# First tile of an attention and two-layer kernel: loads in pieces, no filler matmuls between blocks, another softmax for group 0

## The chip, the cores and the metric

The kernel runs on one core of one Trainium2 chip. The metric is the time of one execution on the device in microseconds (us). TensorE (PE in the profile) multiplies matrices, PEld is its weight load, VectorE is DVE, ScalarE is ACT, GpSimd is POOL, and SyncE (SP) issues the DMAs that bring data from HBM into on-chip memory.

## The reference

The input is a set of attention heads (4 batches, 8 heads, 768 positions, head size 64), each position attending to its own chunk of 32, 16 positions to the left, 8 to the right and 8 memory slots. The result goes through two feed-forward layers.

```python
def _attn_ref(q, k, v, mem_k, mem_v):
    for c in range(nc):                      # 24 chunks of 32
        scores = scale * np.matmul(q_c, k_full.transpose(0, 1, 3, 2))
        scores = scores - np.max(scores, axis=-1, keepdims=True)
        a = np.exp(scores)
        a = a / (np.sum(a, axis=-1, keepdims=True) + 1e-09)
        out[:, :, c_start:c_end] = np.matmul(a, v_full)

def _moe_ref(x, w_in, w_out):                # x is 3072 x 512, d_ff 2048
    h = x @ w_in
    g = np.maximum(0.01 * h, h)
    return g @ w_out

def _moe2_ref(x, w_in, w_out, a, b):
    h = x @ w_in
    P = a[0] + a[1]*h + a[2]*h**2 + a[3]*h**3
    Q = 1.0 + abs(b[0])*abs(h) + abs(b[1])*h**2
    return (P / (Q + 1e-06)) @ w_out
```

All of it is float32. The kernel splits each float32 matrix into a high and a low part and forms three products.

## The kernel before

The 3072 rows are cut into 8 tiles of 384, and each tile into 3 groups of 128. Phase A is attention and the first layer for all tiles, phase B the second layer. In phase A the attention of the next tile is woven into the matmuls of the present one. The first tile has no tile before it, so its three groups run alone at the start of the program, in an order written out by hand for each engine. This stretch, up to `first_gemm1`, is what the diff touches.

For one group, TensorE does `scores` (32 small matmuls, each of which the trace records as two, so 64), then VectorE takes maxima, ScalarE the exponential, TensorE four transpositions (`transpose_probs`), ScalarE copies them out of PSUM (`save_probs_t`), and TensorE does `values` (again 64 records). VectorE then divides by the row sums (`normalise`) and transposes in blocks (`turn_heads`), ScalarE rounds to the high part (`save_heads`) and VectorE forms the low part (`save_heads_low`). `first_gemm1` waits for the high parts of all three groups.

Two ways of doing the softmax exist. `first_exp` (line 653) reads scores from PSUM in eight pieces, each with its own bias, and lets ScalarE sum up each piece; VectorE only gives the maxima and a product for the bias (`first_maxima`). `shift_scores` with `exp_scores` (lines 788 and 649), used in the loop, has VectorE subtract the maxima over all 512 elements, ScalarE take one exponential, and VectorE sum (`sum_rows`).

`keep_warm(n)` issues n matmuls of 384 columns on a zeroed buffer whose result nobody reads. SyncE's program is a list: the q and k part and the v part of groups 0 to 2, the identity, four slices of the first layer's weights, then group 3, then more weights. `load_qk` for a later group waits for `scores_ready`, `load_v` for `heads_ready`, `load_raw` for `w_ready`, which GpSimd raises when it has split a slice (`split_half`). The four `raw` buffers are a ring. The semaphore `heads_ready` counts groups whose `values` are done.

Of the kernel before, what the change touches and what calls it, by code (L numbers as in the profile page):

```python
# [29 lines left out]
ALU = mybir.AluOpType  # L30
# [15 lines left out]
GPT = TILE // P  # L46
# [30 lines left out]
def build(nc, groups, weights, coef, ident_in, out):  # L77
# [166 lines left out]
    def ring(c):  # L244
        return c if c < 3 else c % 2

    def loads(g, c):

        if c < 3:
            return 16  # L250
        return (g - c % 2) * 8 + (16 if c % 2 else 0)

    with nc.Block() as block:

        @block.sync
        def _(sp):

            def load_qk(g, c):
                src = groups[bass.ds(g, 1), :, :].rearrange("a p n -> (a p) n")
                if c >= 3:  # L260
                    sp.wait_ge(scores_ready, g - 1)
                sp.dma_start(grp[ring(c)][:, 0:Q_W + K_W], src[:, 0:Q_W + K_W]).then_inc(qk_loaded[ring(c)], 16)

            def load_v(g, c):
                src = groups[bass.ds(g, 1), :, :].rearrange("a p n -> (a p) n")
                if c >= 3:
                    sp.wait_ge(heads_ready, g - 1)
                sp.dma_start(grp[ring(c)][:, Q_W + K_W:GRP_W], src[:, Q_W + K_W:GRP_W]
                             ).then_inc(v_loaded[ring(c)], 16)

            def load_group(g, c):
                load_qk(g, c)
                load_v(g, c)

            def load_raw(j, r, first=False):

                if not first:
                    sp.wait_ge(w_ready, j - RAW + 1)
                sp.dma_start(raw[:, r, :], weights[bass.ds(j, 1), :, :].rearrange("a p n -> (a p) n")
                             ).then_inc(raw_loaded[r], 16)  # L280
# [39 lines left out]
            sp.sem_inc(y_stored, 1)  # L320


            load_qk(0, 0)
            load_qk(1, 1)
            load_qk(2, 2)
            sp.dma_start(ident[:, :], ident_in).then_inc(ident_loaded, 16)
            for c in range(3):
                load_v(c, c)
            for j in range(RAW):
                load_raw(j, j, first=True)  # L330
            sp.dma_start(cf[:, 0:6], coef).then_inc(coef_loaded, 16)
            load_group(3, 3)
            for j in range(RAW, 2 * RAW):
                load_raw(j, j - RAW)
            load_raw(8, 0)
            load_raw(9, 1)
            load_group(4, 4)
# [100 lines left out]
        def _(pe):  # L438
# [1 line left out]


            def wait_scores(g, c, own_place=False):
                pe.wait_ge(qk_loaded[ring(c)], loads(g, c))
                if not own_place:
                    pe.wait_ge(x_ready, g)

# [16 lines left out]
                last.then_inc(transposed, 1)  # L463

            def wait_values(g, c):
                pe.wait_ge(v_loaded[ring(c)], loads(g, c))
                pe.wait_ge(probs_t_ready, g + 1)

            def values(c, at):
# [12 lines left out]
            def keep_warm(count):  # L482

                for _ in range(count):
                    nc.tensor.matmul(psum[:, H_BANKS[1], 0:TILE], g_hi[:, 0, 0:P], g_hi[:, 0, :], start=True, stop=True)  # L485
# [126 lines left out]
            pe.wait_ge(zeros_ready, 1)  # L612
            keep_warm(13)
            first_scores(0)
            keep_warm(4)
            first_scores(1)
            keep_warm(5)
            first_scores(2)
            keep_warm(2)
            pe.wait_ge(ident_loaded, 16)  # L620
            transpose_probs(0, first_att[0])
            keep_warm(2)
            transpose_probs(1, first_att[1])
            first_values(0)
            first_values(1)
            keep_warm(2)
            transpose_probs(2, first_att[2])
            keep_warm(2)
            first_values(2)
            keep_warm(8)  # L630
            first_gemm1()
            for f in range(1, LAG):
                gemm1(f, f, 0, False)
# [14 lines left out]
        def _(act):  # L648
# [109 lines left out]


            assert GPT == 3  # L760
            first_exp(0, first_att[0])
            first_exp(1, first_att[1])
            save_probs_t(0, first_att[0])
            save_probs_t(1, first_att[1])
# [22 lines left out]
        def _(dve):  # L787
# [15 lines left out]
                                        at.max_v.unsqueeze(3).broadcast_to([P, SETS, CPG, KEYS]),  # L803
                                        ALU.subtract).then_inc(shifted, 1)

            def first_maxima(g, gi, at):

                dve.wait_ge(scores_ready, g + 1)
                if gi == 0:
                    edge = at.scores[:, :, 0, N_MEM:N_MEM + LEFT]  # L810
                    nc.vector.tensor_scalar(edge, edge, NEG, None, ALU.add).then_inc(masked, 1)
                    dve.wait_ge(masked, 1)
                nc.vector.tensor_reduce(at.max_v, at.scores, AX.X, ALU.max).then_inc(maxima_ready, 1)
                dve.wait_ge(maxima_ready, g + 1)
                nc.vector.tensor_scalar(at.safe, at.st[:, 0, :], -SCALE, None, ALU.mult).then_inc(shifted, 1)
# [28 lines left out]
            def turn_heads(g, at):  # L844

                dve.wait_ge(normalised, g + 1)
                nc.vector.transpose(at.heads_t, at.probs).then_inc(turned, 1)
# [102 lines left out]
            nc.vector.memset(g_hi[:, 0, :].bitcast(F32), 0.0).then_inc(zeros_ready, 1)  # L950
            nc.vector.memset(cf[:, 7:8], Q_ONE).then_inc(consts_ready, 1)
            dve.sem_inc(yl_saved, KT)
            for g in range(GPT):
                first_maxima(g, g, first_att[g])
            first_inverses(0, first_att[0])
            first_inverses(1, first_att[1])
            for g in (0, 1):
                normalise(g, first_att[g])
                turn_heads(g, first_att[g])
            first_inverses(2, first_att[2])  # L960
            save_heads_low(0, 0, 0, first_att[0])
            normalise(2, first_att[2])
# [67 lines left out]
```

## Time and profile before

| | us |
|---|---|
| median of 3 runs | 1157.43 |
| lowest, highest | 1156.36, 1158.45 |
| profiled execution, its own time | 1156.13 |
| its span, first to last instruction | 1154.4 |
| TensorE matmuls busy | 1140.4 |
| mean granted TensorE clock | 0.997 |

The span is what the trace covers; 1.73 us of the profiled execution lie outside it. Lines of the trace carry the numbers of this kernel. "Idle before" is the time an engine stood still before an instruction, with what released it; "issue" there means that it waited for nothing that the profile shows. All positions in the trace are counted from the start of the span.

### The profile page before, as it was taken

What the parts mean: (1) busy time and instruction counts of PE and PEld (TensorE: products, weight loads), DVE (VectorE), ACT (ScalarE), POOL (GpSimd) and SP (SyncE); (2) the same over time, 40 slices, a digit from 0 to 9 for tenths busy, and PEclk for the clock granted to TensorE, in tenths of its full rate; (3) what the DMA queues carried; (4) which work ended last, traced back from release to release, by engine and by line L of the source; (5) the groups of instructions that cost most, each with busy time, mean ns of one, the idle gap of its engine ahead of it and who ended that gap; (6) DMA issues with size and microseconds to landing.
All of it is one profiled execution on the core that took longest, in us unless ns stands there. A gap on an engine that the chain in (4) does not pass through costs nothing.

```text
span 1154.4 us, 22877 instructions
## 1 busy us (share of the span) xinstructions
PE 1140.4 (99%) x8966; PEld 1068.7 (93%) x8966; DVE 742.3 (64%) x1384; ACT 568.5 (49%) x1199; POOL 133.3 (12%) x132
## 2 busy tenths in 40 slices
PE   7999999999999999999999999999999999999998
PEld 6999999999999999999999999999999999999996
DVE  4654444544445354444327888888888888888886
ACT  4333223323232232322227676676767667676765
POOL 4981130211202111100000000000000000000000
PEclk8999999999999999999999999999999999999999
DMA  7652534425525254210687010020201002020000
GB/s 267 208 176 87 165 136 141 144 74 183 175 94 186 78 183 157 100 56 2 264 291 246 2 54 30 1 83 1 83 1 66 18 1 83 1 83 1 28 1 28
DMA packets 43016, 114.78 MB, mean 99 GB/s; under 512 B 4896, under 2 KB 5024, under 8 KB 42912
## 3 DMA queue, kind: packets, MB, share of 16 engines
q1 hardware_dynamic: 42912, 113.33, 28.4%
q8 instruction: 72, 1.18, 0.4%
q14 instruction: 32, 0.26, 0.1%
HBM read 77.66 MB, written 35.65 MB: 98 GB/s over the span
## 4 chain that ended last, share of the span: by engine, by line
PE 97%; DVE 1%; ACT 1%; issue 1%; DVEq 0%
PE psum L504 15%; PE psum L506 15%; PE psum L505 15%; PE psum L519 8%; PE psum L538 8%; PE psum L539 8%; PE psum L521 8%; PE psum L520 8%; PE psum L537 7%; PE psum L476 2%; PE psum L453 1%; PE psum L461 1%; PE psum L485 1%; DVE g_lo L862 0%; DVE scratch L859 0%
## 5 line engine op out<-in xcount | busy, mean ns | idle before, releaser
L504 PE MATMUL psum<-x_hi,w_hi 128*128 128x384 f32 x1020 | 342.4, 336 | 1.0 <-DVE x_lo L853 0.8
L506 PE MATMUL psum<-x_hi,w_lo 128*128 128x384 f32 x1020 | 342.6, 336 | 0.0
L505 PE MATMUL psum<-x_lo,w_hi 128*128 128x384 f32 x1020 | 341.6, 335 | 0.0
L859 DVE TENSOR_TENSOR scratch<-psum,scratch 128x384 f32<-128x384 f32 x128 | 71.3, 557 | 235.4 <-ACT scratch L680 234.7
L680 ACT ACTIVATE scratch<-psum 128x384 f32<-128x384 f32 x128 | 62.9, 492 | 277.4 <-PE psum L506 273.5
L504 PEld LDWEIGHTS psum<-x_hi,w_hi 128*128 128x128 f32 x1020 | 191.5, 188 | 7.5 <-issue 1.6
L505 PEld LDWEIGHTS psum<-x_lo,w_hi 128*128 128x128 f32 x1020 | 191.5, 188 | 5.4
L506 PEld LDWEIGHTS psum<-x_hi,w_lo 128*128 128x128 f32 x1020 | 191.4, 188 | 0.0
L519 PE MATMUL psum<-g_hi,w_hi 128*128 128x384 f32 x512 | 177.5, 347 | 0.0
L521 PE MATMUL psum<-g_hi,w_lo 128*128 128x384 f32 x512 | 171.2, 334 | 0.0
L520 PE MATMUL psum<-g_lo,w_hi 128*128 128x384 f32 x512 | 171.2, 334 | 0.0
L539 PE MATMUL psum<-w_hi,g_lo 128*128 128x512 f32 x384 | 152.0, 396 | 0.0
L538 PE MATMUL psum<-w_lo,g_hi 128*128 128x512 f32 x384 | 151.7, 395 | 0.0
L537 PE MATMUL psum<-w_hi,g_hi 128*128 128x512 f32 x384 | 149.5, 389 | 1.5 <-DVE g_lo L868 1.5
L700 ACT ACTIVATE scratch<-psum,cf 128x384 f32<-128x384 f32 x128 | 74.7, 584 | 150.8 <-PE psum L506 150.8
L862 DVE TENSOR_TENSOR g_lo<-scratch,g_hi 128x384 fp32r<-128x384 f32 x128 | 83.7, 654 | 74.2 <-ACT g_hi L686 74.2
L882 DVE SCALAR_TENSOR_TENSOR scratch<-scratch,cf 128x384 f32<-128x384 f32 x128 | 79.1, 618 | 77.8 <-ACT scratch L701 77.8
L686 ACT CAST g_hi<-scratch 128x384 fp32r<-128x384 f32 x128 | 65.7, 513 | 81.8 <-DVE scratch L859 81.8
L519 PEld LDWEIGHTS psum<-g_hi,w_hi 128*128 128x128 f32 x512 | 96.1, 188 | 3.8
L520 PEld LDWEIGHTS psum<-g_lo,w_hi 128*128 128x128 f32 x512 | 96.2, 188 | 0.0
L521 PEld LDWEIGHTS psum<-g_hi,w_lo 128*128 128x128 f32 x512 | 96.1, 188 | 0.0
L539 PEld LDWEIGHTS psum<-w_hi,g_lo 128*128 128x128 f32 x384 | 72.0, 187 | 15.4
(78 smaller groups left out, 1421.7 us busy)
## 6 DMA issues: line engine op xcount, KB each, us to landing
scratch<-groups_in SPq DMA_DIRECT2D x23, 768.0 KB, 4.5
raw<-weights_in SPq DMA_DIRECT2D x64, 256.0 KB, 4.1
scratch<-groups_in SPq DMA_DIRECT2D x23, 512.0 KB, 4.1
w_hi_scratch<-w_high SPq DMA_DIRECT2D x32, 256.0 KB, 4.1
w_lo_scratch<-raw SPq DMA_DIRECT2D x32, 256.0 KB, 4.2
w_hi<-w_hi_scratch SPq DMA_DIRECT2D x32, 256.0 KB, 3.7
w_lo<-w_lo_scratch SPq DMA_DIRECT2D x32, 256.0 KB, 4.6
x_hi_scratch<-x_hi SPq DMA_DIRECT2D x8, 768.0 KB, 3.3
```

The lines of the kernel that those rows point to most:

```text
L504: nc.tensor.matmul(bank, hi, x_hi[:, b, k, :], start=(k == 0), stop=False)
L505: nc.tensor.matmul(bank, hi, x_lo[:, b, k, :], start=False, stop=False)
L506: last = nc.tensor.matmul(bank, lo, x_hi[:, b, k, :], start=False, stop=(k == KT - 1))
L519: nc.tensor.matmul(bank, hi, g_hi[:, f % G_RING, :], start=(f == 0), stop=False)
L520: nc.tensor.matmul(bank, hi, g_lo[:, f % G_RING, :], start=False, stop=False)
L521: last = nc.tensor.matmul(bank, lo, g_hi[:, f % G_RING, :], start=False, stop=(f == NF - 1))
L537: nc.tensor.matmul(bank, hi, w_hi[:, f, 1, :], start=(f == 0), stop=False)
L538: nc.tensor.matmul(bank, hi, w_lo[:, f, 1, :], start=False, stop=False)
L539: last = nc.tensor.matmul(bank, lo, w_hi[:, f, 1, :], start=False, stop=(f == NF - 1))
L700: nc.scalar.activation(absb, h, ACT.Abs, scale=cf[:, 4:5])
L862: nc.vector.tensor_tensor(g_lo[:, f % G_RING, :], leaky[f % 2], g_hi[:, f % G_RING, :].bitcast(F32), ALU.subtract).then_inc(g_lo_ready, 1)
L882: nc.vector.scalar_tensor_tensor(quad[c], h2, cf[:, 6:7], absb, ALU.mult, ALU.add).then_inc(quad_ready, 1)
```

## The change

Three things change in the first tile. The loads of groups 0 to 2 are cut into pieces of 512 columns (2 KB per partition, 256 KB each), and the wait counts of `qk_loaded` and `v_loaded` grow with the number of pieces; slices 4 and 5 of the weights wait until two groups have their `values` done, and group 3, the coefficients and slices 6 and 7 until all three have. The `keep_warm` calls between the attention blocks are gone (17 matmuls), the first one of 13 stays and the last one has 9 instead of 8. Group 0 takes its softmax the way of the loop: difference on VectorE, one exponential on ScalarE, sums on VectorE; the inverses and `normalise` steps are listed anew.

```diff
-    def loads(g, c):
+    def loads(g, c, pieces):
         if c < 3:
-            return 16
-        return (g - c % 2) * 8 + (16 if c % 2 else 0)
+            return 16 * pieces
+        return 16 * (pieces - 1) + (g - c % 2) * 8 + (16 if c % 2 else 0)
...
-            load_qk(0, 0)
-            load_qk(1, 1)
-            load_qk(2, 2)
+            def load_first(c, lo, hi, loaded):
+                for at in range(lo, hi, 512):
+                    sp.dma_start(grp[c][:, at:at + 512], groups[c, :, at:at + 512]).then_inc(loaded[c], 16)
+            for c in range(3):
+                load_first(c, 0, Q_W + K_W, qk_loaded)
             sp.dma_start(ident[:, :], ident_in).then_inc(ident_loaded, 16)
             for c in range(3):
-                load_v(c, c)
+                load_first(c, Q_W + K_W, GRP_W, v_loaded)
             for j in range(RAW):
                 load_raw(j, j, first=True)
+            sp.wait_ge(heads_ready, 2)
+            load_raw(4, 0)
+            load_raw(5, 1)
+            sp.wait_ge(heads_ready, GPT)
+            load_group(3, 3)
             sp.dma_start(cf[:, 0:6], coef).then_inc(coef_loaded, 16)
-            load_group(3, 3)
-            for j in range(RAW, 2 * RAW):
-                load_raw(j, j - RAW)
+            load_raw(6, 2)
+            load_raw(7, 3)
...
             keep_warm(13)
             first_scores(0)
-            keep_warm(4)
             first_scores(1)
-            keep_warm(5)
             first_scores(2)
-            keep_warm(2)
             pe.wait_ge(ident_loaded, 16)
             transpose_probs(0, first_att[0])
-            keep_warm(2)
             transpose_probs(1, first_att[1])
             first_values(0)
             first_values(1)
-            keep_warm(2)
             transpose_probs(2, first_att[2])
-            keep_warm(2)
             first_values(2)
-            keep_warm(8)
+            keep_warm(9)
             first_gemm1()
...
-            first_exp(0, first_att[0])
+            exp_scores(0, first_att[0])
             first_exp(1, first_att[1])
...
-            for g in range(GPT):
-                first_maxima(g, g, first_att[g])
-            first_inverses(0, first_att[0])
+            shift_scores(0, 0, 0, 0, first_att[0])
+            first_maxima(1, first_att[1])
+            sum_rows(0, first_att[0])
+            first_maxima(2, first_att[2])
             first_inverses(1, first_att[1])
```

TensorE, from the start of the program to the first matmul of the first layer: the kernel before, then the changed one.

```order
L485 MATMUL psum<-g_hi 128x384 x12
L453 MATMUL psum<-scratch 32x64 [waits qk_loaded0]
L453 MATMUL psum<-scratch 32x64 x31
L485 MATMUL psum<-g_hi 128x384 x4
L453 MATMUL psum<-scratch 32x64 [waits qk_loaded1]
L453 MATMUL psum<-scratch 32x64 x31
L485 MATMUL psum<-g_hi 128x384 x5
L453 MATMUL psum<-spare 32x64 [waits qk_loaded2]
L453 MATMUL psum<-spare 32x64 x31
L485 MATMUL psum<-g_hi 128x384 x2
L461 MATMUL psum<-ident,scratch 128x128 [waits exp_ready,ident_loaded]
L461 MATMUL psum<-ident,scratch 128x128 x3
```

and the changed one, the same stretch:

```order
L493 MATMUL psum<-g_hi 128x384 x12
L461 MATMUL psum<-scratch 32x64 [waits qk_loaded0]
L461 MATMUL psum<-scratch 32x64 x31
L461 MATMUL psum<-scratch 32x64 [waits qk_loaded1]
L461 MATMUL psum<-scratch 32x64 x31
L461 MATMUL psum<-spare 32x64 [waits qk_loaded2]
L461 MATMUL psum<-spare 32x64 x31
L469 MATMUL psum<-ident,scratch 128x128 [waits exp_ready,ident_loaded]
L469 MATMUL psum<-ident,scratch 128x128 x3
L469 MATMUL psum<-ident,first 128x128 [waits exp_ready]
```

The scores of the three groups now stand back to back, and the transpositions of group 1 follow those of group 0 directly; of the matmuls `L485` (now `L493`) the 13 at the start are left here, and nine stand before the first layer instead of eight.

VectorE, the same stretch of the first tile, before and after (`stats` holds maxima and sums, `scratch` the probabilities of group 0):

```order
L811 TENSOR_SCALAR psum<-psum 128x2x16 [waits scores_ready]
L813 TENSOR_REDUCE stats<-psum 128x8 [waits masked]
L815 TENSOR_SCALAR stats<-stats 128x8 [waits maxima_ready]
L813 TENSOR_REDUCE stats<-psum 128x8 [waits scores_ready]
L815 TENSOR_SCALAR stats<-stats 128x8 [waits maxima_ready]
L813 TENSOR_REDUCE stats<-psum 128x8 [waits scores_ready]
L815 TENSOR_SCALAR stats<-stats 128x8 [waits maxima_ready]
L820 TENSOR_SCALAR stats<-stats 128x8 [waits exp_ready]
L822 RECIPROCAL stats<-stats 128x16 [waits sums_ready]
```

and the changed one:

```order
L799 TENSOR_SCALAR psum<-psum 128x2x16 [waits scores_ready]
L801 TENSOR_REDUCE stats<-psum 128x8 [waits masked]
L804 TENSOR_TENSOR scratch<-psum,stats 128x512 [waits maxima_ready]
L811 TENSOR_REDUCE stats<-psum 128x8 [waits scores_ready]
L813 TENSOR_SCALAR stats<-stats 128x8 [waits maxima_ready]
L826 TENSOR_REDUCE stats<-scratch 128x4x2 [waits exp_ready]
L828 TENSOR_SCALAR stats<-stats 128x8 [waits sums_ready]
L831 RECIPROCAL stats<-stats 128x16 [waits sums_ready]
L811 TENSOR_REDUCE stats<-psum 128x8 [waits scores_ready]
L813 TENSOR_SCALAR stats<-stats 128x8 [waits maxima_ready]
```

Group 0 now gets a difference of 512 elements per partition into `scratch` and, after its exponential, a sum over rows; both moved ahead of the maxima of group 2.

SyncE, the queue of DMA issues from the start, before and after (`raw` are weights, `scratch` and `spare` hold the packed q, k and v of a group):

```order
L262 DMA scratch<-groups_in 128x1536 x2
L262 DMA spare<-groups_in 128x1536
L326 DMA ident<-ident_in 128x128
L268 DMA scratch<-groups_in 128x1024 x2
L268 DMA spare<-groups_in 128x1024
L279 DMA raw<-weights_in 128x512 x4
L331 DMA cf<-coef_in 128x6
L262 DMA scratch<-groups_in 128x1536 [waits scores_ready]
L268 DMA scratch<-groups_in 128x1024 [waits heads_ready]
L279 DMA raw<-weights_in 128x512 [waits w_ready] x6
```

and the changed one:

```order
L326 DMA scratch<-groups_in 128x512 x6
L326 DMA spare<-groups_in 128x512 x3
L330 DMA ident<-ident_in 128x128
L326 DMA scratch<-groups_in 128x512 x4
L326 DMA spare<-groups_in 128x512 x2
L279 DMA raw<-weights_in 128x512 x4
L279 DMA raw<-weights_in 128x512 [waits w_ready,heads_ready]
L279 DMA raw<-weights_in 128x512 [waits w_ready]
L262 DMA scratch<-groups_in 128x1536 [waits scores_ready,heads_ready]
L268 DMA scratch<-groups_in 128x1024 [waits heads_ready]
L340 DMA cf<-coef_in 128x6
L279 DMA raw<-weights_in 128x512 [waits w_ready] x4
```

The first three groups come in 15 issues of 512 columns instead of six. The fifth slice of weights now waits for `heads_ready` and stands ahead of group 3, whose `scores_ready` wait was alone before and now stands with `heads_ready`.

## Rows read from the trace of the kernel before

**Rows 1.** The page: busy time of each engine, share, instructions.

```profile
PE 1140.4 (99%) x8966; PEld 1068.7 (93%) x8966; DVE 742.3 (64%) x1384; ACT 568.5 (49%) x1199; POOL 133.3 (12%) x132
```

**Rows 2.** Chain that ended last, 0 to 29: start, length, what.

```profile
7.46 2.48 ACT scratch L659 x16
9.94 2.38 ACT first L659 x16
15.48 3.89 issue
```

**Rows 3.** Timeline of TensorE, 0 to 29: start, length, engine, line, operation, releaser.

```profile
12.36 0.33 PE L461 MATMUL psum<-ident,first 128*128 128x128 f32 x1 [1.17 <-ACT first L659]
13.35 0.55 PE L461 MATMUL psum<-ident,first 128*128 128x128 f32 x3 [0.66 <-issue]
14.66 0.81 PE L476 MATMUL psum<-scratch,first 64*32 64x64 f32 x60
19.37 0.42 PE L476 MATMUL psum<-scratch,first 64*32 64x64 f32 x4 [3.89 <-issue]
22.35 1.17 PE L476 MATMUL psum<-spare,scratch 64*32 64x64 f32 x64
23.45 2.52 PE L485 MATMUL psum<-g_hi 128*128 128x384 f32 x8
25.81 0.40 PE L596 MATMUL psum<-x_hi,w_hi 128*128 128x384 f32 x1
28.26 0.34 PE L504 MATMUL psum<-x_hi,w_hi 128*128 128x384 f32 x1
```

**Rows 4.** Timeline of VectorE, 5 to 27.

```profile
8.71 0.17 DVE L815 TENSOR_SCALAR stats<-stats 128x8 f32<-128x8 f32 x1
23.56 0.69 DVE L840 TENSOR_TENSOR first<-psum,stats 128x512 f32<-128x512 f32 x1
```

**Rows 5.** Timeline of ScalarE, 5 to 29.

```profile
12.10 0.68 ACT L667 COPY scratch<-psum 128x512 f32<-128x512 f32 x1
25.03 0.62 ACT L674 CAST x_hi<-scratch 128x512 fp32r<-128x512 f32 x1 [2.31 <-DVE scratch L847]
```

**Rows 6.** Line 651, the exponential of later groups: durations ns min/median/max.

```profile
L651 ACT ACTIVATE scratch<-scratch x3: 630/632/633, 39.8 to 78.3; 128x512 f32<-128x512 f32 x3
```

**Rows 7.** Line 802, the difference of later groups, same columns.

```profile
L802 DVE TENSOR_TENSOR scratch<-psum,stats x3: 691/691/692, 39.1 to 77.6; 128x512 f32<-128x512 f32 x3
```

**Rows 8.** DMA queues, 10.9 to 11: packets, MB, share of 16 engines.

```profile
q8 instruction: 1, 0.02, 65.7%
```

**Rows 9.** DMA queues, 17 to 17.1.

```profile
q8 instruction: 1, 0.02, 69.0%
```

**Rows 10.** Stretches: length, engines busy, granted clock (last but two), DMA share, GB/s.

```profile
15.48:18.50 3.02, 0.00 (x0) 0.00 (x0) 0.68 (x1) 1.93 (x11) 2.85 (x4) 1.00 0.48 189
18.50:25.33 6.83, 5.83 (x82) 4.92 (x83) 5.35 (x8) 1.41 (x3) 5.02 (x7) 0.50 0.66 218
3.00:6.00 3.00, 3.00 (x70) 2.75 (x72) 0.00 (x0) 0.00 (x0) 0.00 (x0) 1.00 1.01 412
12.50:14.50 2.00, 1.34 (x68) 0.98 (x67) 0.34 (x2) 0.85 (x3) 0.00 (x0) 1.00 1.05 397
```

**Rows 11.** Timeline of GpSimd, 15 to 30.

```profile
15.88 1.27 POOL L416 TENSOR_TENSOR w_lo<-raw,w_hi 128x512 fp32r<-128x512 f32 x1
24.53 0.62 POOL L413 TENSOR_SCALAR w_hi<-raw 128x512 fp32r<-128x512 f32 x1 [1.56 <-DMA raw<-weights_in]
```

**Rows 12.** Timeline of the DMA issues of SyncE, 0 to 40.

```profile
0.82 0.87 SPq L262 DMA_DIRECT2D scratch<-groups_in  x2
7.97 0.33 SPq L262 DMA_DIRECT2D scratch<-groups_in  x1
20.21 9.39 SPq L279 DMA_DIRECT2D raw<-weights_in  x6
```

More of the change, by code:

```diff
@@ L442, in wait_scores @@
             def wait_scores(g, c, own_place=False):
-                pe.wait_ge(qk_loaded[ring(c)], loads(g, c))
+                pe.wait_ge(qk_loaded[ring(c)], loads(g, c, (Q_W + K_W) // 512))
                 if not own_place:
@@ L465, in wait_values @@
             def wait_values(g, c):
-                pe.wait_ge(v_loaded[ring(c)], loads(g, c))
+                pe.wait_ge(v_loaded[ring(c)], loads(g, c, V_W // 512))
                 pe.wait_ge(probs_t_ready, g + 1)
@@ L804, in shift_scores, with first_maxima @@
                                         ALU.subtract).then_inc(shifted, 1)
-            def first_maxima(g, gi, at):
+            def first_maxima(g, at):
                 dve.wait_ge(scores_ready, g + 1)
[L809 to L812, printed above, removed]
                 nc.vector.tensor_reduce(at.max_v, at.scores, AX.X, ALU.max).then_inc(maxima_ready, 1)
@@ L952, in _ @@
             dve.sem_inc(yl_saved, KT)
-            for g in range(GPT):
-                first_maxima(g, g, first_att[g])
-            first_inverses(0, first_att[0])
+            shift_scores(0, 0, 0, 0, first_att[0])
+            first_maxima(1, first_att[1])
+            sum_rows(0, first_att[0])
+            first_maxima(2, first_att[2])
             first_inverses(1, first_att[1])
-            for g in (0, 1):
-                normalise(g, first_att[g])
-                turn_heads(g, first_att[g])
+            normalise(0, first_att[0])
+            turn_heads(0, first_att[0])
+            normalise(1, first_att[1])
+            turn_heads(1, first_att[1])
             first_inverses(2, first_att[2])
```

## The prediction

> **What bounds the kernel now.** I read the page first. TensorE is busy 99% of the span [rows 1], so outside a few places nothing can be gained except by starting its real work sooner. The first tile is such a place: nothing is there for TensorE until attention has made x. The timeline of TensorE comes next, and it shows the first matmul of the first layer at 25.81 [rows 3]. From there on it has hardly a gap, so what the changed kernel wins or loses is how much earlier or later that matmul stands, plus what the clock takes from the matmuls behind it.
>
> The chain of waits says what fills the 25.81 us. ScalarE's exponentials of groups 0 and 1 are on it for 2.48 and 2.38 us, and one piece of 3.89 us called "issue" is on it [rows 2]. That piece lies between the 60th and the 61st of 64 equal small matmuls of `values` of group 1, none of which waits for a semaphore; a shorter one of 0.66 us lies between the first and second transposition of group 1 [rows 3]. Between the two stops stand 3 + 64 + 60 = 127 matmuls and as many weight loads, about 254 instructions. The instruction queue begins a packet of 0.02 MB between 10.9 and 11.0 and the next between 17.0 and 17.1 [rows 8, 9], each 2.4 us ahead of the end of a stop, 13.35 and 19.37. I read this as TensorE running out of code: a block of some 256 instructions is fetched by DMA, and the fetch stood behind the loads of data. DMA share is 1.01 to 1.05 in the stretches from 3 to 6 and 12.5 to 14.5 [rows 10].
>
> The Trainium skill, in "Runtime: NRT & Kernel Launch", section "Instruction fetch mechanics", says that code comes in blocks of 16 KB and that crossing a block's edge is mostly hidden. The block size agrees with the trace; that it is hidden does not, with 3.89 us in the open. By that rule only ScalarE's part of the sum below would be won, and the changed kernel would take 1156.4.
>
> After the long stop the granted clock is 0.50 of full speed from 18.50 to 25.33, 1.2 instead of 2.4 GHz, and 1.00 before [rows 10]. TensorE stood still from 15.48 to 19.37 before and while it fell; stops of 1.17 and 0.66 us did not bring it down. It rose 5.96 us after work began again, with few gaps. At the low level 64 small matmuls take 1.17 us, where 60 took 0.81 before, so 0.86 for 64; matmuls of 384 columns take about 0.35 instead of some 0.18 us each (12 of them stand between 25.81 and 28.26, a short wait among them, and eight mostly at the low level took 2.52) [rows 3].
>
> **The change, part by part.**
>
> *Softmax of group 0.* On VectorE the product of 0.17 us becomes a difference of 0.69 [rows 4, 7], so ScalarE begins 0.52 later than 7.46, at 7.98, but its one exponential takes 0.63 instead of 2.48 [rows 2, 6]. It is free at 8.61. Group 1 is ready at 8.71 + 0.17 = 8.88 [rows 4] and its 2.38 us run from 8.92 to 11.30 instead of 9.94 to 12.32: 1.02 us earlier. The row sums, about 0.7 us more on VectorE by the difference's price, fall in its idle time before group 2 has scores and cost nothing; if they did push group 2's maxima by a whole 0.7, these would still be ready by 11.5, and ScalarE takes group 2 only after 12.
>
> *After that, without code waits.* ScalarE copies group 0's transposed probabilities (0.6 to 0.68 [rows 5]) and, after 0.6 us of transpositions, group 1's: it is free at about 12.6 and does group 2's exponentials until 12.6 + 2.4 = 15.0. Transpositions of group 2 to 15.6; ScalarE rounds group 0 (0.62 [rows 5]) beside them and copies to 16.3; `values` of group 2 takes 0.86, to 17.2. In the kernel before this ended at 23.52, and VectorE's `normalise` of group 2 began at 23.56, 2.25 us ahead of 25.81 [rows 3, 4]. With the same 2.25 the first matmul would stand at 19.5: 6.3 us earlier is the upper end.
>
> *Code fetches.* Without the fillers the stops move. Ahead of the first stop stand 13+64+4+64+5+64+2+4+2+1 = 223 matmuls; in the changed order 213 of these remain by the end of group 1's transpositions, so the edge falls after 10 matmuls of `values` of group 0, at about 12.1. The next edge is 127 further: 64 + 64 + 4, minus the 10 done, leaves it 5 matmuls into `values` of group 2. If the blocks come when they came before, at 13.35 and 19.37 [rows 3], `values` of group 2 would end at 20.2 and the first matmul stand at 22.5: 3.3 us earlier, the lower end. I take both blocks earlier. The q, k and v loads are now 2 KB per row, so that what is queued in front of a fetch is shorter, and group 3's q and k, 768 KB issued at 7.97 [rows 12], are out of the way. What is left is 3 x 1280 + 64 + 4 x 256 KB = 5.0 MB; at 412 GB/s that is 12.2 us, and from a start of the flow near 2.5 it ends at about 14.7. A fetch asked for near 13 is then served by 15 and usable 2.4 us later, as the two before. So the second edge opens at about 17.3, `values` of group 2 ends at 18.1, and 18.15 + 2.25 = 20.4. The term is 25.8 - 20.4 = 5.4 us, ScalarE's 1.02 in it.
>
> *Rate of the loads.* Stretches with 6 KB rows move 412 GB/s, with 2 KB rows 397 [rows 10], 4% less: 0.1 us on the first 768 KB, which is on the path, and 0.3 by the end of q and k, which is not. SyncE issues 15 DMAs where it issued six, each about 0.44 us (two in 0.87 [rows 12]); 256 KB per 0.44 us is above what the DMA engines move. I take 0.1. The Trainium skill, "DMA: Bandwidth & Descriptors", "Measured (HBM→SBUF, 128 partitions, SWDGE, issued from GpSimd)", advises batches of 1 MiB or more for 75% of peak; 256 KB pieces would fall below. By that rule the first group would land at least 0.6 us later and the sum would be smaller by 0.5. The 256 KB weight loads at 397 GB/s speak against it.
>
> *Fillers and the clock.* The 17 removed matmuls cost at most 17 x 0.18 = 3 us of TensorE's own time, nearly all in idle time, so removing them gives nothing by itself. They kept TensorE busy, and now idle stretches of some 0.7 to 1.5 us stand between the blocks, five or six of them by the times above. Each is far shorter than 3.89, but they come one after the other. Lower end of the clock's cost: 0, it stays high. Upper end: it is low from early on. Then small blocks add 0.3 each (two on the path, 0.6), the nine fillers behind `values` take 9 x 0.35 = 3.2 instead of 1.6, ending about 0.6 after the rest is ready, and the clock rises 6 us after work gets dense (17.3), at 23.3, so that real matmuls from 21.6 to 23.3 lose half of 1.7, 0.85. With 0.4 for transpositions that is 2.5. I take 1.2, the middle, since no row shows such a spacing.
>
> *Weights.* GpSimd has the first slice ready at 15.88 + 1.27 = 17.15, and its matmul runs at 25.81 [rows 3, 11]: 8.7 us to spare, 3 after the change. Each later slice takes it 1.9 us, each later block of 12 matmuls takes TensorE 2.1. Slice 4 was late (1.56 us [rows 11]) since it was issued after 20.21 behind 512 KB of v [rows 12]; now it is issued when slice 0 is split, near 17.2, and comes by 19.8, so that GpSimd gains 1.6. Slices 6 and 7 stand behind group 3, issued near 19; they land by 25 and are wanted at 27. Cost 0; if that cover is gone, TensorE waits us for us. Group 3 itself lands near 23.5, wanted at about 29.
>
> *Sum.* 5.4 - 0.1 - 1.2 = 4.1 us off the profiled execution: 1156.13 (span 1154.4 and 1.7 around it) becomes 1152.0. The median of the runs is 1.3 above that execution, so the forecast for a median is 1157.43 - 4.1 = 1153.3.
>
> **The rivals.**
>
> A. The clock stays high and the code is there: 5.4 to 6.2 us, 1151.6. For it: 1.17 and 0.66 us of idleness did not lower the clock. Against: no row has so many stops in a row.
>
> B. The clock falls early and stays low into the first layer: 5.4 - 0.1 - 2.5 = 2.8 at least, and with a later rise or a code wait in part 1.5; 1155.3. For it: the 5.96 us that it took to rise.
>
> C. The code wait comes back at full length in `values` of group 2, since a fetch waits for whatever is queued and the four weight slices still are: 3.3 - 0.1 - 1.2 = 2.0, 1155.4. For it: TensorE entered a block at 13.35 and the next one's packet began only at 17.0, 3.6 us later. Against: less data is in front of it.
>
> D. Slower than before: the fillers' removal leaves the first layer itself at 1.2 GHz. Place: the matmuls behind `first_gemm1`; price: 0.17 us each (0.35 against 0.18). The gain of 5.3, less 1.3 for the low clock ahead of them, is used up after 24 matmuls, two output blocks, and 1159.8 is reached after 38. Against it: these matmuls have no gaps once weights are there, and dense work raised the clock in 6 us.
>
> **How the numbers follow.** Forecast 0.45, A 0.2, B 0.18, C 0.12, D 0.05. What a measurement can tell from no change is about 0.2%, 2.3 us: faster means below 1155.1. The forecast's own range is 1152.0 to 1154.6, all faster; A is faster; B and C are so 4 times in 10. That is 0.45 + 0.2 + 0.12 = 0.77 faster, 0.19 the same, 0.04 slower. The range that leaves out no more than 2 in 10 runs from 1150.8, the upper end of A, to 1155.9, most of B and C.
>
> **What would show it.** The difference of group 0 near 7.25 and ScalarE's group 1 from 8.9; stops called "issue" 10 matmuls into `values` of group 0 and 5 into `values` of group 2, the second under 1 us; data quiet between 15 and 17; the first matmul of the first layer near 20.4 to 21.5; a low-clock stretch of under 6 us around it. It would be wrong if the fetch packets start as late as before, if TensorE waits for GpSimd's weights in the first tile, or if matmuls of 384 columns come 0.35 us apart beyond 25.

## The result, and the profile after

| | before | changed |
|---|---|---|
| median of 9 runs each, us | 1157.28 | 1153.78 |
| lowest, highest | 1155.98, 1159.37 | 1150.58, 1155.56 |
| profiled execution, span | 1156.13, 1154.4 | 1152.93, 1151.1 |

The ratio is 0.9970, with a 95% interval of 0.9962 to 0.9978: 3.5 us faster, give or take 0.9. The forecast was 4.1 us.

The page of the changed kernel, its line of engines, answers to [rows 1]:

```profile
PE 1136.9 (99%) x8950; PEld 1066.0 (93%) x8950; DVE 741.6 (64%) x1385; ACT 565.9 (49%) x1184; POOL 132.6 (12%) x132
```

TensorE's timeline in the first tile answers to [rows 3]; lines have moved, 461 is `scores`, 469 the transpositions, 484 `values`, 493 the fillers, 604 the first matmul of the first layer.

```profile
5.85 0.86 PE L461 MATMUL psum<-scratch 64*32 64x64 f32 x64 [0.64 <-DMA scratch<-groups_in]
7.82 0.86 PE L461 MATMUL psum<-scratch 64*32 64x64 f32 x64 [1.11 <-DMA scratch<-groups_in]
9.88 0.86 PE L461 MATMUL psum<-spare 64*32 64x64 f32 x64 [1.19 <-DMA spare<-groups_in]
12.18 0.66 PE L469 MATMUL psum<-ident,first 128*128 128x128 f32 x4 [0.86 <-ACT first L661]
12.77 0.32 PE L484 MATMUL psum<-scratch 64*32 64x64 f32 x9
14.23 0.87 PE L484 MATMUL psum<-scratch 64*32 64x64 f32 x53 [1.15 <-issue]
16.01 1.11 PE L469 MATMUL psum<-ident,first 128*128 128x128 f32 x4
17.97 1.41 PE L484 MATMUL psum<-spare,scratch 64*32 64x64 f32 x64 [0.85 <-ACT scratch L669]
19.31 2.77 PE L493 MATMUL psum<-g_hi 128*128 128x384 f32 x9
21.92 0.34 PE L604 MATMUL psum<-x_hi,w_hi 128*128 128x384 f32 x1
```

The first layer starts at 21.92 instead of 25.81, 3.9 us earlier; of this 3.3 are left in the spans (1151.1 against 1154.4). The stop called "issue" stands behind 9 matmuls of `values` of group 0 and is 1.15 us long; the trace lists no second one, where [rows 3] had 3.89 us inside `values` of group 1. But the scores of the three groups start at 5.85, 7.82 and 9.88, where they stood at 5.40, 7.09 and 9.01 before: the loads are later. Group 2's transpositions take 1.11 us and its `values` 1.41, both at the low clock. The same 64 matmuls took 1.17 at the low clock in [rows 3], so some 0.2 us may be what is left of the second stop; the trace does not single it out.

The chain that ended last, answering to [rows 2]: start, length, what.

```profile
3.16 4.62 DMA scratch<-groups_in
9.65 2.48 ACT first L661 x16
13.08 1.15 issue
```

In place of ScalarE's exponentials of group 0 a DMA now stands at the head of the chain, the last piece of q and k of group 1. Stretches, answering to [rows 10]:

```profile
3.00:6.00 3.00, 2.36 (x27) 2.04 (x34) 0.00 (x0) 0.00 (x0) 0.00 (x0) 1.00 0.91 319
14.50:21.40 6.90, 6.05 (x189) 5.25 (x166) 5.75 (x10) 3.56 (x14) 5.09 (x6) 0.51 0.37 121
```

The flow of the first loads is 319 GB/s where it was 412, and the granted clock is 0.51 from 14.5 to 21.4. VectorE's difference and ScalarE's exponential take what was forecast, 0.69 and 0.63 us, though they start 0.46 and 0.45 later than forecast:

```profile
7.71 0.69 DVE L804 TENSOR_TENSOR scratch<-psum,stats 128x512 f32<-128x512 f32 x1
```

```profile
8.43 0.63 ACT L653 ACTIVATE scratch<-scratch 128x512 f32<-128x512 f32 x1 [6.41 <-DVE scratch L804]
```

GpSimd's first split starts at 16.06, 0.9 us later than before. TensorE nowhere waits for GpSimd:

```profile
16.06 0.62 POOL L421 TENSOR_SCALAR w_hi<-raw 128x512 fp32r<-128x512 f32 x1 [15.61 <-DMA raw<-weights_in]
```

### The profile page after: what moved, and what is told of

It is laid out like the page before. It is cut to its first block, busy times and chain, and to the rows that moved or that the text cites. A ratio compares the mean times of both kernels' runs of the same rounds, so it can differ in the third digit from the quotient of the medians.

```text
span 1151.1 us, 22841 instructions
## 1 busy us (share of the span) xinstructions
PE 1136.9 (99%) x8950; PEld 1066.0 (93%) x8950; DVE 741.6 (64%) x1385; ACT 565.9 (49%) x1184; POOL 132.6 (12%) x132
## 4 chain that ended last, share of the span: by engine, by line
PE 95%; DVE 2%; ACT 1%; issue 1%; DMA 0%; SPq 0%; DVEq 0%
PE psum L512 15%; PE psum L514 15%; PE psum L513 15%; PE psum L527 8%; PE psum L546 8%; PE psum L547 8%; PE psum L545 8%; PE psum L528 7%; PE psum L529 7%; PE psum L484 2%; PE psum L461 1%; PE psum L469 1%; DVE g_lo L860 1%; DVE scratch L857 0%; ACT g_hi L688 0%
```

## The experiments

Each ratio is against runs of the kernel before on the same chip, with its 95% interval; the last column is the ratio's distance from 1 times 1157. The intervals reach 0.9 to 1.7 us to each side; rows whose intervals overlap are not told apart by their ratios.

| kernel | loads | held back | fillers between | softmax of group 0 | ratio (95%) | us |
|---|---|---|---|---|---|---|
| changed | pieces | yes | none | new | 0.9970 (0.9962 to 0.9978) | -3.5 |
| e1 | whole | yes | none | new | 0.9947 (0.9932 to 0.9961) | -6.1 |
| e12, the same again | whole | yes | none | new | 0.9952 (0.9939 to 0.9966) | -5.6 |
| e2 | pieces | yes | old | old | 0.9988 (0.9978 to 0.9997) | -1.4 |
| e3 | whole | no | none | old | 0.9972 (0.9964 to 0.9981) | -3.2 |
| e4 | whole | no | old | new | 0.9992 (0.9983 to 1.0000) | -0.9 |
| e5 | whole | no | none | new | 0.9970 (0.9960 to 0.9981) | -3.5 |
| e6 | pieces | no | none | new | 0.9979 (0.9969 to 0.9988) | -2.4 |
| e7 | q, k whole, v pieces | yes | none | new | 0.9963 (0.9949 to 0.9976) | -4.3 |
| e8 | whole | yes | two of six | new | 0.9970 (0.9960 to 0.9981) | -3.5 |
| e9 | whole | yes | none, 9 more in front | new | 0.9972 (0.9962 to 0.9981) | -3.2 |
| e10 | whole | yes | two, longer ones | new | 0.9956 (0.9942 to 0.9970) | -5.1 |
| e11 | q, k in two pieces | yes | none | new | 0.9967 (0.9955 to 0.9980) | -3.8 |

Two theories stood at the start. In theory 1 what matters is how much data is queued in front of a code fetch, and the pieces merely delay the data. In theory 2 the pieces let the code through.

**e1: whole loads.**

```diff
-            for c in range(3):
-                load_first(c, 0, Q_W + K_W, qk_loaded)
+            load_qk(0, 0)
+            load_qk(1, 1)
+            load_qk(2, 2)
             sp.dma_start(ident[:, :], ident_in).then_inc(ident_loaded, 16)
             for c in range(3):
-                load_first(c, Q_W + K_W, GRP_W, v_loaded)
+                load_v(c, c)
```

> The changed kernel with the first three groups loaded whole again (six issues), the held-back order, the missing fillers and the new softmax kept. Theory 1 (pieces only delay the data; what shortens the code wait is what is queued, not the size of a piece): scores of group 0 to 2 stand at 5.4, 7.1 and 9.0 as in the kernel before, first matmul of the first layer 0.7 us earlier than the changed kernel's 21.9, code wait in values of group 0 up to 1.2 us longer but hidden in part; time 0.3 to 0.8 us below the changed kernel. Theory 2 (2 KB pieces let the code fetch through): the fetch packets start later than in the changed kernel by 1 us or more, a wait called issue of 2 us or more in values of group 0 or group 2, time above the changed kernel by 1 us or more.

Measured: 1150.45 us, against 1157.01 for the kernel before. The gain is larger than either theory allowed, and theory 2 is out: without pieces the code came earlier, not later. The instruction queue's packets begin at 10.8 and 15.0 here and at 11.8 and 15.7 in the changed kernel. Timeline of TensorE in e1:

```profile
5.22 0.86 PE L457 MATMUL psum<-scratch 64*32 64x64 f32 x64
7.10 0.86 PE L457 MATMUL psum<-scratch 64*32 64x64 f32 x64 [1.02 <-DMA scratch<-groups_in]
9.01 0.86 PE L457 MATMUL psum<-spare 64*32 64x64 f32 x64 [1.05 <-DMA spare<-groups_in]
13.33 1.09 PE L480 MATMUL psum<-scratch 64*32 64x64 f32 x54 [0.40 <-issue]
17.50 1.30 PE L480 MATMUL psum<-spare,scratch 64*32 64x64 f32 x64 [0.77 <-ACT scratch L665]
21.77 0.41 PE L600 MATMUL psum<-x_hi,w_hi 128*128 128x384 f32 x1
```

The scores are back at 5.2, 7.1 and 9.0, the code wait is 0.40 us, and again none is listed in `values` of group 2. Against the changed kernel that is 2.7 us by the ratios (2.1 with e12, whose interval overlaps the changed kernel's a little). Only 0.15 of it shows at the first matmul of the first layer in these two profiles (21.77 against 21.92); e1's profile had the low clock for longer, from 11.1. At group 3's transpositions it is 0.8 (35.41 against 36.19). Behind that, the changed kernel's TensorE has waits that e1's has not: 0.30 and 0.31 us for VectorE's low part of x at 50.11 and 69.75, and 0.27 for ScalarE at 353.74. Each profile also has one longer wait for a low part of x, early in one and late in the other, which cancels. In the changed kernel and in e1:

```profile
125.67 0.41 PE L512 MATMUL psum<-x_hi,w_hi 128*128 128x384 f32 x1 [0.86 <-DVE x_lo L851]
```

```profile
439.08 0.41 PE L508 MATMUL psum<-x_hi,w_hi 128*128 128x384 f32 x1 [0.78 <-DVE x_lo L847]
```

**e2 to e4: one part each.** e2 puts the new loads alone into the kernel before, e3 takes out the fillers alone, e4 changes the softmax alone. Their edits are the respective hunks of the change.

> The kernel before with the new loads alone (pieces and held-back order). If the code wait of 3.89 us is a fetch behind queued data, and less is queued: the wait stays between the 60th and 61st matmul of values of group 1 but shrinks to 2 us or less; scores come 0.5 to 0.9 us later; time 1 to 2 us below the kernel before. If the wait has nothing to do with the queued data: it stays 3.9 us, and the time is 0.5 to 1 us above the kernel before.

Measured 1155.80, ratio 0.9988. As expected the wait stayed at its instruction and shrank, to 1.97 us. The scores came 1.0, 1.2 and 1.4 us later than before, more than expected and more than in the changed kernel.

```profile
18.61 0.43 PE L484 MATMUL psum<-scratch,first 64*32 64x64 f32 x4 [1.97 <-issue]
```

> The kernel before with the fillers between blocks taken out alone (9 in front of the first layer). The edges of the code blocks move to 10 matmuls into values of group 0 and 5 into values of group 2. If data in front sets the wait: the second block still comes near 19.4 and TensorE waits about 1 to 2 us for it, first matmul of the first layer 1.5 to 2.5 us earlier than 25.8; granted clock low by then. If the clock is what fillers were for: the clock stays low further into the first layer and the time is the same or 1 us above the kernel before.

Measured 1153.75, ratio 0.9972: 3.2 us from this part alone, not told apart from the whole gain of the change. The wait moved into `values` of group 2, behind its fourth matmul, and is 1.11 us:

```profile
17.98 0.30 PE L476 MATMUL psum<-spare,scratch 64*32 64x64 f32 x4 [0.77 <-ACT scratch L661]
19.39 1.14 PE L476 MATMUL psum<-spare,scratch 64*32 64x64 f32 x60 [1.11 <-issue]
23.50 0.52 PE L596 MATMUL psum<-x_hi,w_hi 128*128 128x384 f32 x1
```

The block of code came at 19.39, where it came at 19.37 before. It is the place of the wait that changed: in the kernel before all of group 2's transpositions and `values` stood behind it, here only 60 matmuls of group 2 and the nine fillers. The first layer starts at 23.50, 2.3 us earlier, at the low clock at first.

> The kernel before with only group 0's softmax changed. ScalarE's exponentials of group 1 start 1.0 us earlier; but the second code block is asked for only after TensorE has entered the one before and comes behind the same data, so if the code wait bounds the tile, it starts earlier and grows: the wait becomes 4.5 us or so, end still near 19.4, and the time is within 0.5 us of the kernel before. If ScalarE bounds the tile: 1.0 us below.

Measured 1155.99, ratio 0.9992, 0.9 us with an interval from 0 to 2.0. Neither branch held as written: the wait did not grow, it stayed 3.89 us, and its end moved by 0.13 us only. The profile is of the slowest of the 11 executions (1157.77), so it cannot show where the median won its 0.9.

```profile
14.53 0.81 PE L476 MATMUL psum<-scratch,first 64*32 64x64 f32 x60
19.24 0.30 PE L476 MATMUL psum<-scratch,first 64*32 64x64 f32 x4 [3.89 <-issue]
```

The three parts add to 1.4 + 3.2 + 0.9 = 5.5 us; together they give 3.5. The loads and the fillers both work on the same wait, which would explain a smaller sum; but each figure is good to about 1 us only, so the difference of 2.0 is barely clear of noise. The softmax adds least: e5, which has it, and e3, which has not, are otherwise the same kernel and 0.2 us apart, no difference.

**e5 and e6: nothing held back.** e5 is e1, e6 the changed kernel, each with group 3 and the coefficients right behind the first four slices of weights:

```diff
-            sp.wait_ge(heads_ready, 2)
-            load_raw(4, 0)
-            load_raw(5, 1)
-            sp.wait_ge(heads_ready, GPT)
-            load_group(3, 3)
             sp.dma_start(cf[:, 0:6], coef).then_inc(coef_loaded, 16)
-            load_raw(6, 2)
-            load_raw(7, 3)
+            load_group(3, 3)
+            for j in range(RAW, 2 * RAW):
+                load_raw(j, j - RAW)
```

> The kernel before with the missing fillers and the new softmax, its loads unchanged: whole, and group 3 and the weights in their old order. It differs from e1 (1150.45) only in that nothing is held back. If what is queued in front sets the code wait: the second code packet starts near 17.0 instead of 15.0, TensorE waits about 2 us in values of group 2, and the time is 1.5 to 2.5 us above e1, 1152 to 1153. If holding back is worth nothing: 1150.5, the same as e1.

> The changed kernel with its pieces, but nothing held back: group 3 and the coefficients right behind the first four slices of weights. If what is queued sets the code wait: second packet near 17.5, a wait of about 2 us in values of group 2, time 1 to 2 us above the changed kernel (1153.8). If pieces alone let the code through: no such wait, and the time is the changed kernel's.

e5 took 1152.62 (0.9970) and e6 1153.49 (0.9979). The second packet of the instruction queue began at 16.8 in e5, and at 15.0 in e1. The queues' view of the stretch 16.8 to 16.9 in e5:

```profile
q8 instruction: 1, 0.02, 68.9%
```

and of 15.0 to 15.1 in e1:

```profile
q8 instruction: 1, 0.02, 59.9%
```

In e5 TensorE then waited 1.32 us behind the fourth matmul of `values` of group 2:

```profile
17.62 0.42 PE L476 MATMUL psum<-spare,scratch 64*32 64x64 f32 x4 [0.77 <-ACT scratch L661]
19.37 1.14 PE L476 MATMUL psum<-spare,scratch 64*32 64x64 f32 x60 [1.32 <-issue]
```

Holding back is worth 2.7 us between e5 and e1, on the same chip; five of e1's six executions are below all eight of e5's. With e12 for e1 it is 2.1. With pieces (e6 to the changed kernel) it is 1.0 us, and the intervals overlap, so there it is not resolved, though e6's profile has the wait (1.52 us) that the changed kernel lacks.

The start of the second packet sorts all the runs by their loads, whatever their fillers and softmax:

| loads | held back | second packet begins, us |
|---|---|---|
| whole | no (before, e3, e4, e5) | 16.7 to 17.0 |
| whole, or only v cut | yes (e1, e7, e8, e9, e10, e12) | 14.6 to 15.0 |
| q and k cut | yes (changed, e2, e11) | 15.7 to 16.2 |
| q and k cut | no (e6) | 17.9 |

And wherever the trace shows a second stop, it ends 2.4 to 2.6 us behind that packet's start: 16.2 and 18.61 in e2, 17.0 and 19.39 in e3, 15.0 and 17.60 in e12, 17.9 and 20.45 in e6. TensorE entered the block before at nearly the same time in e1 and e5 (13.33 and 13.39), so the 1.8 us between their packets come from what is queued.

**e7 and e11: how finely the loads are cut.** e7 leaves q and k whole and cuts v, e11 cuts q and k in two:

```diff
-                for at in range(lo, hi, 512):
+                for at in range(lo, hi, width):      # 768 for q and k, 512 for v
```

> The changed kernel with q and k of groups 0 to 2 loaded whole and v still in two pieces each. If the pieces cost time because the first loads flow at 319 instead of 412 GB/s: scores at 5.4, 7.1 and 9.0, as in e1, and the time is e1's 1150.5 within 0.6. If pieces anywhere in front of the weights cost: weights still late (GpSimd starts after 15.6) and the time lies half way, 1152.

> The changed kernel with q and k in two pieces of 768 columns instead of three of 512; v still in pieces of 512. If the slower flow of the first loads comes from the number of issues: 3 to 6 us moves 350 to 380 GB/s (319 with three pieces, 412 with one), first scores at 5.5 to 5.7, and a time between e1 and the changed kernel, about 1.5 us below the changed one. If any cutting costs the whole: scores at 5.85 and the changed kernel's time.

e7 took 1151.29 (0.9963), with scores at 5.4, 7.3 and 9.2. Its time lies between e1's and the changed kernel's and is told apart from neither. e11 took 1152.32 (0.9967), with scores at 5.8, 8.1 and 10.1; that is the changed kernel's time, against the branch that expected 1.5 us less. e11's flow from 3 to 6:

```profile
3.00:6.00 3.00, 3.00 (x25) 2.56 (x32) 0.00 (x0) 0.00 (x0) 0.00 (x0) 1.00 0.95 362
```

So 412, 362 and 319 GB/s for one, two and three issues of q and k. The figure for whole loads is steady (408 to 420 in ten profiles); the one for three issues is not: e6 has 300 and e2 270 with the same loads. From 6 to 9 the order is not kept either: the changed kernel has 376 and e11 341. The cut of the first loads delays the scores; what each cut is worth in time is resolved only between e1 and the changed kernel. The same rows of 2 KB flow at 403 GB/s from 9 to 12 in the changed kernel, and at 397 in [rows 10], so it is not the size of a row alone. The slow flow is in the first microseconds of the loads; why, no run here tells.

**e8 to e10 and e12: fillers, the edge and the clock.** e8 puts back the fillers behind the scores of groups 0 and 1.

```diff
             first_scores(0)
+            keep_warm(4)
             first_scores(1)
+            keep_warm(5)
             first_scores(2)
```

> e1 (whole loads) with the fillers behind the scores of groups 0 and 1 (4 and 5 matmuls) put back, none later. In e1's profile the granted clock was low from 11.1 to 21.4. If the missing fillers cost through the clock: it stays high past 11 and falls later or not at all, and the median is 0.3 to 1.5 us below e1's 1150.45. If the clock falls only with the later idle stretches: no difference beyond 0.3.

Measured 1152.70, ratio 0.9970: slower than e1 by 2.7 us, against both branches. The granted clock stayed high until 18.3. But:

```profile
17.13 0.66 PE L465 MATMUL psum<-ident,first 128*128 128x128 f32 x4 [2.62 <-issue]
```

Nine more matmuls in front had moved the edge of the code block from 4 matmuls inside `values` of group 2 to just ahead of the group's transpositions, where ScalarE and VectorE still need the result. e9 tests that by itself: it is e1 with three of its 13 leading fillers cut into twelve short ones:

```diff
-            keep_warm(13)
+            keep_warm(10)
+            for _ in range(12):
+                nc.tensor.matmul(psum[:, H_BANKS[1], 0:96], g_hi[:, 0, 0:P], g_hi[:, 0, 0:96], start=True, stop=True)
```

> e1 (whole loads, held back, no fillers between blocks) with three of the 13 leading fillers cut into twelve of a quarter of the columns: nothing is added between the blocks, but nine more matmuls stand in front, so the edge of the second code block moves from 4 matmuls into values of group 2 to just ahead of group 2's transpositions, where it was in e8. If the place of the edge is what cost e8 its 3 us against e1: a wait called issue of 1.5 to 2.7 us ahead of the transpositions of group 2, and a time 1.5 to 3 us above e1. If e8 lost them by the fillers' own time or by the clock: no such wait and e1's time within 0.5 us.

Measured 1152.92, ratio 0.9972, against 1150.52 for the same kernel without the nine instructions on the same chip (e12): 2.3 us for nine more idle matmuls, though no more columns, in front of everything. Ten of e9's 11 executions are above all five of e12's.

```profile
9.05 0.86 PE L457 MATMUL psum<-spare 64*32 64x64 f32 x64 [1.11 <-DMA spare<-groups_in]
17.38 0.66 PE L465 MATMUL psum<-ident,first 128*128 128x128 f32 x4 [2.05 <-issue]
```

The wait of 2.05 us is where it was predicted. The longer lead-in did delay something by itself: group 0's scores start at 6.32, against 5.78 in e12, and group 1's transpositions at 12.24 against 11.70. But group 2's scores stand at 9.05, as in e1, and the 0.5 us are covered by the wait, whose end, 17.38, follows the packet of 14.9 by 2.5.

e10 restores the fillers with fewer, longer instructions:

```diff
-            keep_warm(13)
+            keep_warm_long(10)          # 512 columns each
             first_scores(0)
+            keep_warm_long(3)
             first_scores(1)
+            keep_warm_long(4)
```

> e1 with fillers of 512 columns: 10 in front (as many columns as 13 of 384), 3 behind the scores of group 0 and 4 behind those of group 1. Only 4 matmuls more stand in front, so the second edge stays inside or at the start of values of group 2. If the clock costs e1 something and the edge is what spoilt e8: clock high beyond 11, no code wait ahead of group 2's transpositions, time 0.3 to 1.2 us below e1. If the clock costs nothing: e1 within 0.3. If fillers cost by themselves: above e1.

> e1 once more, on the chip of e9 to e11, as their base: 5.5 to 6.5 us below the kernel before if the first figure holds; 3.5 to 4.5 if the first comparison was lucky in its chip or in the clock's phase.

e10 took 1149.93 (0.9956), e12 1150.52 (0.9952): no difference, whichever figure is taken. The edge shows in e10 only as a wait of 1.34 us ahead of `values` of group 2, put down to ScalarE, where the other runs wait 0.77 for the same copy. The clock was never low in e10's profile nor, this time, in e12's, so that e1 and e12 compare the two clocks in one program. They are single executions on two chips, and executions of one program differ by some 1 us, so what counts is where the two traces meet. Stretch 11.1 to 21.4, e1 first:

```profile
11.10:21.40 10.30, 8.47 (x208) 7.12 (x209) 7.21 (x12) 5.87 (x25) 5.99 (x6) 0.50 0.58 199
```

and e12:

```profile
11.10:21.40 10.30, 6.58 (x213) 5.34 (x214) 7.94 (x13) 6.22 (x26) 5.90 (x6) 1.00 0.56 197
```

The first matmul of the first layer stands at 21.77 in e1 and 20.69 in e12, 1.1 us apart. It is not more since TensorE, at the high clock, reaches the edges of the code blocks sooner: e12 has stops of 0.23 and 0.46 us where e1 had 0.40 and none. The two executions took 1150.66 and 1150.52 us. In e12, TensorE had given the time back by group 3's transpositions, 0.64 of it in this wait:

```profile
20.69 0.41 PE L600 MATMUL psum<-x_hi,w_hi 128*128 128x384 f32 x1 [0.51 <-ACT x_hi L672]
35.39 0.66 PE L465 MATMUL psum<-ident,scratch 128*128 128x128 f32 x4 [0.64 <-ACT scratch L649]
```

In e1 the same instruction stood at 35.41 and waited for nothing, and in e7, whose first layer starts at 21.00, it stood at 35.40:

```profile
35.40 0.66 PE L469 MATMUL psum<-ident,scratch 128*128 128x128 f32 x4 [0.41 <-ACT scratch L653]
```

Three starts of the first layer, up to 1.1 us apart, end at one place. ScalarE waits there for VectorE, which begins group 3's maxima at 33.29 in e1 and 33.27 in e12. VectorE did not gain from the earlier start: its first `g_lo` took 1.48 us in e12 and 0.77 in e1 (start, length):

```profile
25.05 1.48 DVE L856 TENSOR_TENSOR g_lo<-scratch,g_hi 128x384 fp32r<-128x384 f32 x1 [0.58 <-ACT g_hi L684]
```

```profile
25.79 0.77 DVE L856 TENSOR_TENSOR g_lo<-scratch,g_hi 128x384 fp32r<-128x384 f32 x1 [0.58 <-ACT g_hi L684]
```

The executions of the kernel before say the same in the large: of the 29 on e1's chip, the five with a mean granted clock of 0.995 average 1157.3 us and the seven with 0.999 average 1156.8. By estimate that 0.004 is some 9 us more at half clock, for 0.5 us that are within the noise.

## Why the prediction was right, and where it was not

The time (1153.8 for 1153.3) and the direction were right, and the main mechanism, TensorE running out of code, was the right one. Two of the three terms were not, and that the sum came out is in part luck.

- *Softmax of group 0.* The durations were right, 0.69 and 0.63 us. The 1.02 us at ScalarE did not reach the end: group 1's exponentials began at 9.65 and not 8.92, since its scores were late, and e3 and e5 differ by 0.2 us.
- *The edges.* Right: the stop came behind 9 matmuls of `values` of group 0 for the 10 counted, and the next edge 4 or 5 matmuls into `values` of group 2 (e3, e5, e12). The sum had the price too: with the blocks arriving as late as before, it put the gain of the moved edges at 3.3 us, and e3, where the block still arrives at 19.4, measures 3.2. Only the sentence that removing the fillers "gives nothing by itself" misleads: it holds for their own time, not for the edges that they move. A wait for code costs by what stands behind it, as e9 shows with the sign turned.
- *The code fetches.* Both blocks were to come earlier than before. The first came later: its packet began at 11.8 instead of 10.9, and the stop ended at 14.23 instead of 13.35. The second packet began at 15.7, so that its code was there near 18.1 and not 17.3; it was hardly waited for, since `values` of group 2 began only at 17.97. Of the two causes named, group 3's loads out of the way is the one that the runs support (e5 against e1). Shorter rows are not: with whole loads the packets started at 10.8 and 15.0, earlier than with pieces.
- *Rate of the loads.* This step failed: 0.1 us was taken and the scores came 0.45, 0.73 and 0.87 us late. The rate of 2 KB rows was read from a stretch in which the queue was long full. Whole loads are 2.1 to 2.7 us faster (e12, e1) than the pieces. About 0.8 of this was seen by 35 us into the span. The rest lies in short later waits, and why they are there was not isolated. The rule of the Trainium skill cited in the prediction ("DMA: Bandwidth & Descriptors", "Measured (HBM→SBUF, 128 partitions, SWDGE, issued from GpSimd)"), larger batches, stood on the right side. The prediction's estimate by it was at least 0.6 us later for the first group; the traces agree, since e1's scores began at 5.22 without waiting for a load and the changed kernel's waited for theirs until 5.85. They do not agree with 1 MiB as the mark: the whole loads of 768 KB are below it too, and ran at 412 GB/s.
- *The clock.* 1.2 us was taken. The clock fell, at 14.5, and was low for 6.9 us, more than the "under 6" of the forecast. Between e1 and e12 it moves the first layer's start by 1.1 us, but by 35.4 nothing is left of it: VectorE was next. So this term was too large by about 1 us, and the loads' term too small by 2.0 to 2.6. Without the loads' term the forecast is 4.2 us; e1 and e12, which leave the pieces out, measure 6.1 and 5.6. The rest of the change won 1.4 to 1.9 us more than forecast and the pieces lost it again: that is the luck in the sum.
- *Rivals.* A, the clock high and the code there, is nearly what e10 and e12 show, with whole loads: 5.1 and 5.6 us. B and D needed the low clock in the first layer; it ended at 21.4, before the first matmul at 21.92. The price that D put on such matmuls is real: in e3's profile, where the low clock lasts longer, they start 0.32 us apart instead of 0.17. C, a code wait in `values` of group 2, is what e6 shows when nothing is held back, at 1.52 us and a gain of 2.4.

## What to carry to other kernels

Where TensorE stops inside a run of equal instructions and waits for nothing, count the instructions to the next such stop and look for a packet of the instruction queue ahead of the end of each. If the distances agree (127 matmuls and their weight loads here, and 2.4 to 2.6 us from packet to work), it is out of code. The stop can then be shortened by queueing less data in front of the fetch, and it can be moved, by a few instructions more or fewer ahead of it, to a place where nothing waits behind it; a filler costs not only its time but its place in the code. Cut the first loads of a program no finer than their use demands, and read a rate from the stretch in which it will be used.

## What the runs showed of the hardware that was not expected

- First loads cut into 2 KB rows ran at 270 to 319 GB/s from 3 to 6 us (e2, e6, changed) and at 403 from 9 to 12 (changed); whole 6 KB rows ran at 408 to 420 in the same first stretch.
- Nine more idle matmuls in front of the program's work, with no more columns, cost 2.3 us (e9 against e12) through the place of a code block's edge.
- The packet of a code block began 1.8 us later with 768 KB more of data issued ahead of it (16.8 in e5, 15.0 in e1), and its code was in use 2.4 to 2.6 us behind the packet's start in every run with a visible stop.
- 10 us at half clock in front of a chain of other engines put the first layer 1.1 us later (e1 against e12); at 35.4 us the two traces stand at the same instruction within 0.02.
